# An attention and two-layer MoE kernel: moving the first pair's memory product, its scaling and the gate arithmetic

## The reference

```python
scores = scale * q @ k.T                      # per head, causal mask
a = exp(scores - max); a /= a.sum(-1) + 1e-9
local = a @ v
q_p = where(q > 0, q, exp(q) - 1) + 1         # phi
mem_out = (q_p @ M_prev) / (q_p @ z_prev + 1e-6)
g = sigmoid(beta)                             # one gate per head
x = g * mem_out + (1 - g) * local
```

## Time and profile before

| | us |
|---|---|
| time, median of 3 executions | 325.53 |
| lowest and highest | 324.82 and 326.0 |
| the profiled execution: time | 326.0 |
| the profiled execution: span in the trace | 324.2 |
| PE busy | 309.2 (95%) |
| DVE busy | 204.6 (63%) |
| ACT busy | 143.9 (44%) |
| POOL busy | 146.1 (45%) |

### The profile page before, as it was taken

The page is one execution under the profiler, slowest core; times in us unless marked ns, Lnnn a source line. Parts: engine busy times, 40 slices in busy tenths (PEclk is TensorE's granted clock), DMA queues, the critical chain, the costliest instruction groups (busy, mean ns, idle before and its releaser), DMA issues.

```text
span 324.2 us, 7041 instructions
## 1 busy us (share of the span) xinstructions
PE 309.2 (95%) x2725; PEld 251.4 (78%) x2725; DVE 204.6 (63%) x540; ACT 143.9 (44%) x318; POOL 146.1 (45%) x170
## 2 busy tenths in 40 slices
PE   7979999999999999989999999999999999999991
PEld 6556676676677988858999989898998877756681
DVE  5879998999975556686856378377665623522300
ACT  1776766766965235544533343354334222002020
POOL 4767997998998100915850031603430070700301
PEclk9999999999999999999999999999999999999998
DMA  8989866861456500000003139420140192059940
GB/s 161 177 194 217 217 174 103 204 172 38 134 163 141 173 0 2 2 0 2 0 2 54 20 145 371 78 38 3 21 76 16 23 418 80 3 166 398 398 153 10
DMA packets 76056, 38.48 MB, mean 119 GB/s; under 512 B 67026, under 2 KB 67034, under 8 KB 74996
## 3 DMA queue, kind: packets, MB, share of 16 engines
q1 hardware_dynamic: 72580, 36.76, 40.5%
q10 hardware_dynamic: 2416, 0.59, 0.9%
q0 software_dynamic: 1024, 0.64, 0.7%
HBM read 32.66 MB, written 5.43 MB: 117 GB/s over the span
## 4 chain that ended last, share of the span: by engine, by line
PE 90%; DVE 4%; POOL 2%; issue 2%; ACT 0%; POOLq 0%; DVEq 0%
PE bank_a L1686 15%; PE bank_b L1686 15%; PE bank_out L1643 6%; PE bank_a L1544 4%; PE bank_pt L1745 4%; PE bank_pt L1596 4%; PE bank_b L1745 4%; PE bank_a L1620 3%; PE bank_b L1897 3%; PE bank_b L1906 3%; PE bank_a L1897 2%; PE bank_a L1906 2%; PE bank_out L1719 2%; PE bank_out L1640 2%; PE bank_b L1539 2%
## 5 line engine op out<-in xcount | busy, mean ns | idle before, releaser
L677 POOL TENSOR_SCALAR prob<-prob,rl,gate_loc 128x512 f32<-128x512 f32 (+3 forms) x64 | 41.7, 666 | 13.5 <-DVE rl L1140 13.5
L1686 PE MATMUL bank_a<-x_hi,win_hi 128*128 128x288 f32 x128 | 39.2, 307 | 0.0
L1686 PE MATMUL bank_b<-x_hi,win_hi 128*128 128x288 f32 x128 | 38.1, 298 | 0.0
L1686 PE MATMUL bank_a<-x_lo,win_hi 128*128 128x288 f32 x128 | 37.8, 295 | 0.0
L1686 PE MATMUL bank_b<-x_lo,win_hi 128*128 128x288 f32 x128 | 37.7, 295 | 0.0
L1686 PE MATMUL bank_a<-x_hi,win_lo 128*128 128x288 f32 x128 | 37.7, 294 | 0.0
L1686 PE MATMUL bank_b<-x_hi,win_lo 128*128 128x288 f32 x128 | 37.6, 294 | 0.0
L855 ACT ACTIVATE prob<-prob,negmax 128x512 f32<-128x512 f32 (+3 forms) x64 | 35.1, 555 | 1.0 <-DVE negmax L1090 1.0
L761 POOL DMA_INDIRECT few_d<-row,slot_l x12 | 12.7, 1062 | 49.4 <-DVE jobs_f L1364 38.1
L919 ACT ACTIVATE g_raw<-bank_a,biases 128x576 f32<-128x576 f32 x16 | 11.9, 744 | 51.9 <-DVE sq L1214 51.9
L706 POOL TENSOR_TENSOR x_lo<-xT,x_hi 128x1152 fp32r<-128x1152 f32 x4 | 11.3, 2816 | 47.5 <-ACT x_hi L868 47.5
(11 more groups left out here) (300 smaller groups left out, 764.1 us busy)
## 6 DMA issues: line engine op xcount, KB each, us to landing
w_sb<-in_moe_w_dram SPq DMA_DIRECT2D x6, 2048.0 KB, 12.6
win_raw<-in_moe_w_in_dram SPq DMA_DIRECT2D x4, 1024.0 KB, 5.6
wout<-in_moe_w_out_dram SPq DMA_DIRECT2D x4, 1024.0 KB, 6.2
win_raw<-in_moe_w_in_dram SPq DMA_DIRECT2D x1, 4096.0 KB, 14.0
out_dram<-zero_row SPq DMA_DIRECT2D x8, 288.0 KB
x_d<-x_rows SPq DMA_DIRECT2D x32, 72.0 KB
v_sb<-in_v_dram SPq DMA_DIRECT2D x16, 128.0 KB, 2.4
qn<-in_q_dram SPq DMA_DIRECT2D x24, 72.0 KB, 4.8
```

The source lines that it names most:

```text
L677: pool.tensor_scalar(prob[u][:, h, :], prob[u][:, h, :], rl[:, c:c + 1], gate_loc[:, 2 * j + h:2 * j + h + 1], ALU.mult, ALU.mult).then_in ...
L1686: last = pe.matmul(h_bank(d)[:, t, :], w[:, m, f:f + P], x[c % 2][:, m, :], start=(m == 0 and n == 0), stop=(m == KT - 1 and n == 2))
```

## The change

Five moves, and no operation is added or removed. On GpSimd, `gates()` goes behind the two phi operations of pair 0. On VectorE, `gates()` goes behind the row maxima of tiles 3 and 2 of pair 0; `scale_memory(0)` goes from the end of round 0 to round 1, behind `row_factor(1, 0)` and ahead of `phi(1)`; `turn_k(2)` goes from behind `copy_pt(0, 6)` to ahead of it. On TensorE, `memory(0)` goes from the end of round 0 to round 1, behind `scores(1, 2)`.

```diff
--- before.py
+++ after.py
@@ -719,11 +719,11 @@
             pool.wait_ge(s_gates, 1)
             pool.tensor_scalar(gate_inv[:, :], gate_mem[:, :], 1.0, None, ALU.add).then_inc(s_gates, 1)
             tail_block(0)
-            gates()
             pool.wait_ge(s_exq, 1)
             pool.tensor_scalar(qpT[1][:, :], qT[0][:, :], 0.0, None, ALU.max).then_inc(s_above, 1)
             pool.wait_ge(s_above, 1)
             pool.tensor_tensor(qpT[0][:, :], qpT[0][:, :], qpT[1][:, :], ALU.add).then_inc(s_phi, 1)
+            gates()
             for r in range(NPAIR + 1):
                 if r > 0:
                     scale_prob(r - 1, 1, 0)
@@ -1159,7 +1159,6 @@
             copy_k(1)
             dve.wait_ge(s_tail, 3)
             row_max(0, 4)
-            scale_memory(0)
 
             for r in range(1, NPAIR + 1):
                 j = r - 1
@@ -1182,10 +1181,10 @@
                     row_max(r, 0)
                     row_factor(r, 0)
                 if r == 1:
+                    scale_memory(0)
                     phi(1)
+                    turn_k(2)
                 copy_pt(j, 6)
-                if r == 1:
-                    turn_k(2)
                 if r < NPAIR:
                     row_max(r, 4)
                 if r < NPAIR - 1:
@@ -1815,6 +1814,8 @@
                     scores(r, 2)
                     if r == 0:
                         turn_q(1)
+                    if r == 1:
+                        memory(0)
                 else:
                     pe.wait_ge(s_wlo, KT)
                     pe.wait_ge(s_mn, NPAIR)
@@ -1845,7 +1846,6 @@
                     memory(r)
                 if r == 0:
                     turn_k(1)
-                    memory(0)
                 if r > 0:
                     last_values(j)
```

## The result

The changed kernel takes 328.44 us (median of 5, 328.16 to 329.6) against 325.53 us before (5, 324.82 to 326.36). The ratio is 1.0097, 95% interval 1.0069 to 1.0124: slower by 2.9 us between the medians and by 3.1 us between the means. The profiled execution took 327.87 us, its span is 326.1 us. The forecast was +1.8 us, 327.3 us, range 325.7 to 328.4: right sign, too small a size.

What follows compares the result with a forecast made beforehand. TensorE bounds the kernel (90% of the chain), so the start of add_memory(0) decides: 25.14 to about 26.95 through VectorE's queue, despite TensorE's 0.6 us gain. +1.8 on 326.0 gives 327.8; against the 325.53 median, 327.3 us, range 325.7 to 328.4.

Steps and rivals of the forecast that it cites:

- The gates behind phi: GpSimd, pair 0: gates lose their cover behind phi, first scale at 14.75 instead of 14.47, +0.28 us on GpSimd.
- The row factor was feared to collide with the gates on GpSimd: VectorE's small row-factor operation, 166 ns median, 1391 worst, might wait for one gate operation at a shared port; sum unchanged.
- `memory(0)` on TensorE: Round 1: its 1.46 us moves behind scores(1, 2); scores(1, 3) at 16.82, TensorE ready for add_memory(0) 0.6 us earlier.
- `scale_memory(0)` on VectorE: Round 1: ends at 26.91 in VectorE's queue, so add_memory(0) starts at 26.95, +1.8 us, with TensorE idle 2.4 us.
- the third rival's second half: TensorE behind the 2.4 us pause: clock lost, 5.1 us of work could double, 332.4 us; chance 2%.
- `turn_k(2)`: VectorE, ahead of copy_pt(0, 6): both results come before TensorE needs them, so the swap costs nothing.
- the rounds behind: Rounds after the delayed start: as long as before, 12.01 us each, all shifted by 1.8 us.

Runs made afterwards that it cites:

- e5: Kernel before with only the two gates() moved, on GpSimd and VectorE, as in the change: 324.18 us against 324.43 for before.
- e6: Changed kernel with scale_memory(0) ahead of copy_pt(0, 3) and both gates() back in their old places: 323.29 us against 324.43 for before.
- e1: Changed kernel with only scale_memory(0) moved earlier, behind row_factor(0, 1) and ahead of copy_pt(0, 3): 323.53 us against 324.33 for before.
- e3: Kernel before with only scale_memory(0) moved late, to round 1 ahead of phi(1): 327.94 us against 324.33 for before.
- e4: The changed kernel again, no edit, timed against the kernel before on one chip: 327.59 us against 324.33.
- e8: Changed kernel with turn_k(2) back behind copy_pt(0, 6): 327.73 us against 324.43 for before, ratio 1.0066.
- e7: Changed kernel with scale_memory(0) moved earlier, right behind copy_pt(0, 5): 324.06 us against 324.43 for before.
- e2: Changed kernel with 16 unused identity transposes on TensorE ahead of values(0), filling its pause: 325.81 us, ratio to before 1.0042.
- e9: Kernel before with 7 unused identity transposes on TensorE between turn_prob(0, 4) and turn_prob(0, 5): 325.31 us against 325.49 for before.

## Why the prediction was wrong, step by step

- **The gates behind phi**: first scale forecast at 14.75, measured 14.66. In the kernel before that is hidden behind `memory(0)` (e5); in the changed kernel it is not, and costs about 0.26 us (e6 against e1), as the forecast's 0.28 had it. The row factor was feared to collide with the gates on GpSimd. It started at 13.94, while the first gate operation ran (13.85 to 14.06), and took 0.17 us; that operation took 0.21 us (0.20 before): no collision.
- **`memory(0)` on TensorE**: `scores(1, 3)` forecast 16.82, measured 16.84; TensorE ready for `add_memory(0)` 0.6 us earlier by the forecast, 0.5 in e1, where nothing else holds it.
- **`scale_memory(0)` on VectorE**: `add_memory(0)` forecast 26.95, measured 26.92; pause forecast 2.4 us, measured 2.19 by the view's modelled ends. This was the mechanism, and e3 shows that this move alone brings the whole loss.
- **The step that failed** is the third rival's second half, "if the 2.4 us pause cost TensorE its clock", with a chance of 2%. The sum had no term for it. It belonged into it as a term of 1.67 us (half clock for 3.4 us), not of 5.1. I had dismissed it by the earlier trace rows, where the clock is still 1.00 up to 4 us after the last work. That row was misread, and it was the wrong place to stop. The next window of the same trace has the fall:

```profile
322.00:324.00 2.00, 0.00 (x0) 0.00 (x0) 0.00 (x0) 0.00 (x0) 0.00 (x0) 0.52 0.04 8
```

It comes at about 322.1 us, 4.5 us after TensorE's last work (317.5). In the traces the fall follows the start of a pause by 2.2 us (e4), 3.0 (e5, from the first of its two waits), 3.2 (e3), 3.7 (the changed kernel and e8) and 4.5 us (the end of before), whether work has begun again by then or not. So a full clock inside a pause, or 4 us after it began, says nothing of what the pause will cost. No window of before has work behind a pause of that length, so its trace could give the fall but not its price. The Trainium skill, "TensorE: Matmul & The Clock Gate", section "What's actually happening", has the gate set by how busy the array has been recently; the trace agrees as to the two levels, 1.00 and 0.50. This rule should have had a price and a fair chance.
- **The reference itself**: in 26 of the 72 runs of before in the experiments the clock group is the lower one, and the means of the two groups differ by 1.2, 1.3 and 1.4 us on the three chips. So before loses on average up to 0.5 us (26/72 of 1.3), most likely to the same cause, and the difference to the changed kernel is smaller by that. On the chip of e4 the changed kernel's mean is 3.3 us above the mean of before's upper group and 3.0 us above the mean of all its runs; the traces have 3.28 to 3.45.
- **`turn_k(2)`** and the rounds behind: no cost, 12.01 us a round, as forecast.

## What to carry to other kernels

When a change makes TensorE wait for about two microseconds in the middle of a busy stretch (1.8 and 2.2 us here), put two terms in the sum: the wait, and a stretch at half clock behind it. Look for the second in the microseconds after the pause, not in the pause, and over several executions, since with shorter waits close together it struck in some and spared others. And before an operation leaves a place, look at whether that place is a gap: here 1.28 us of VectorE work left a gap and went to a place where VectorE's queue had no time left; in the gap ahead of `copy_pt(0, 3)` (e1) the kernel gained instead of lost.

## What the hardware showed unexpectedly

- The clock fell 1.5 us after TensorE had resumed (1.4 in e3, at once in e4), which is 2.2 to 3.7 us after the pause began, and stayed at half for about 3.4 us although TensorE was busy all the time.
- Behind one wait of 0.83 us (e7) or 0.46 us (e2) it did not fall in the profiled executions, and none of the 24 runs has a mean clock under 0.993; behind 1.81 us (e3) and 2.2 us (the change, e4, e8) it fell in all profiled executions; with two waits of 0.67 and 1.04 us close together it fell in the profiled execution of e5 and not in that of before, whose waits are the same.
- Idle-looking filler work has a use: 7 transposes whose result nobody reads went with no slower group of executions in 12 runs (e9), and 16 of them took 1.78 us off the changed kernel (e2).
